# Nine output projections in three rounded passes, and fourteen middle taps added by DMA

## The chip, the cores and the metric

The kernel runs on one core of a Trainium2 chip. The metric is the device time of one execution in microseconds. Its engines are TensorE (PE; its weight loads are PEld), VectorE (DVE), ScalarE (ACT), GpSimd (POOL) and SyncE (SP), each with a queue of its own that it works through in order. They meet through semaphores.

## What is computed

A batch of 4 sequences of 1088 tokens goes through attention with a product of two sketches, then through a layer that mixes by a Fourier transform and has a small feed-forward part (layer 1), and then through layer 2, where the change is:

```python
h = np.maximum(x @ w_in, 0.0)                      # 128 -> 1024
hp = pad(h, 1, axis=1)
conv_out = sum(conv_w[k] * hp[:, k:k + S, :] for k in range(3))
gate = 1.0 / (1.0 + np.exp(-conv_out))
return h * gate @ w_out                            # 1024 -> 128
```

## The kernel before

Everything is fp32. Layer 2 keeps tokens in the free dimension: a chunk is one batch (of 4) and 128 of the 1024 hidden channels (of 8), so there are NI = 32 chunks, numbered i = 0 to 31 here, each 128 partitions by 1088 tokens. PSUM holds a chunk in three tiles of 364 columns.

A chunk goes through these steps, each on the engine that is named:

- `hidden(i)`, PE, L521 to L523: for each of three tiles, x times w_in in three passes. An fp32 value is split into a rounded high half (type fp32r) and the rest, the low half, and low x high, high x low and high x high are summed. The halves of x come from layer 1 (`x2hi`, `x2lo`).
- `relu(i)`, ACT, L792: three copies with relu from PSUM to `h2`, a ring of HIDDENS = 5 buffers. It waits for the product of chunk i - 5.
- `left_tap(i)` (L1056) and `right_tap(i)` (L1061), DVE: gate = ratio0 * left + middle, then gate = ratio1 * right + gate. The taps are scaled so that the middle one is 1; the sigmoid puts the scale back.
- `sigmoid(i)`, ACT, L798, in place in `gate`.
- `product(i)`, DVE, L1068: gate = h2 * gate.
- `project(i)`, PE, L600: three matmuls in fp32 with w_out (`wout`), which add up the eight chunks of a batch in three PSUM banks. `output(b)` (ACT, L807) copies them out after the eighth.

The order on each queue is written out. PE does hidden(i), then slots of layer 1, then the projections up to i + 1 - lag(i); `LAGS` sets how many chunks projection stays behind, 6 to 8. DVE does in its turn i left tap i, product i - 2 and right tap i. ACT does in its turn i relu i + 1, output if one is due, and sigmoid i - 1. Into all three a `slot(n)` of layer 1 is put where `PACES` says: up and down matmuls (L561 and others) on PE, `hidden_high` (L736) and `mixed_high` (L741) on ACT, low halves on DVE. The slots end at chunk 22. GpSimd works out the ten reciprocal deviations of layer 1 and has nothing to do later.

```python
LAGS = ((-1, 6), (15, 7), (19, 8), (24, 7), (26, 6), (28, 5), (30, 4))
def projected(i):
    return max(0, i + 1 - lag(i))
```

## Time and profile before

| | us |
|---|---|
| median of 3 runs | 256.98 (256.5 to 289.55) |
| the profiled execution | 256.51 |
| its span, first to last instruction | 254.7 |
| PE busy in it | 247.2 |
| DVE busy in it | 220.2 |
| ACT busy in it | 157.0 |

The span leaves out 1.8 us of the profiled execution's time that lie before the first and behind the last instruction. Busy time is the union of an engine's instructions; overlapping instructions of one engine count once.

### The profile page before, as it was taken

Reading aid. Unit: us, or ns where it says so; the run is one execution under the profiler, and the core shown is the slowest. Engines: PE = TensorE matmul, PEld = TensorE weight load, DVE = VectorE, ACT = ScalarE, POOL = GpSimd, SP = SyncE. Lnnn points to the kernel's source line nnn. Section 1 sums busy time; section 2 is a strip of 40 time slices with the busy share of each in tenths; the row PEclk is TensorE's granted clock in tenths of the full one; section 3 lists DMA queues with packets and bytes.
Section 4 is the critical chain, followed back from the end, with each engine's and each line's share of the span. In section 5 each row is a group of like instructions: output and inputs, shape, how many; then the busy total and the mean of one; then the engine's idle time right before and its main releaser. Section 6 shows DMA issues by size and latency. Waiting matters only on the chain.

```text
span 254.7 us, 4283 instructions
## 1 busy us (share of the span) xinstructions
PE 247.2 (97%) x1522; PEld 210.7 (83%) x1522; DVE 220.2 (86%) x404; ACT 157.0 (62%) x325; POOL 28.4 (11%) x90
## 2 busy tenths in 40 slices
PE   8999999999999999989999999999999999999995
PEld 7999999998989999978887777778778777777752
DVE  0847888899998688897799999999979999997992
ACT  2351733333586547688997766769769576667552
POOL 0000000001603343575200000000000000000000
PEclk9999999999999999999999999999999999999999
DMA  7959730300000000000000000002000002002002
GB/s 249 349 217 348 307 98 0 97 4 0 3 0 1 3 1 0 3 3 3 0 0 3 0 0 0 3 0 89 0 0 3 1 0 87 3 0 87 0 0 88
DMA packets 4340, 13.04 MB, mean 51 GB/s; under 512 B 736, under 2 KB 1504, under 8 KB 4320
## 3 DMA queue, kind: packets, MB, share of 16 engines
q1 hardware_dynamic: 4176, 12.74, 13.7%
q8 instruction: 12, 0.20, 0.3%
q14 instruction: 8, 0.07, 0.1%
q10 hardware_dynamic: 144, 0.03, 0.1%
HBM read 10.54 MB, written 2.23 MB: 50 GB/s over the span
## 4 chain that ended last, share of the span: by engine, by line
PE 46%; DVE 5%; ACT 3%; issue 2%; ACTq 0%
PE ps L600 20%; PE ps L521 7%; PE ps L523 7%; PE ps L522 7%; PE ps L561 5%; DVE arena L1061 2%; DVE arena L1056 1%; ACT arena L722 1%; ACT arena L798 1%; PE ps L552 1%; DVE arena L1068 1%; PE ps L531 0%; DVE x_nat L970 0%; DVE arena L977 0%; DVE x2lo L1004 0%
## 5 line engine op out<-in xcount | busy, mean ns | idle before, releaser
L600 PE MATMUL ps<-arena,wout 128*128 128x364 f32 (+1 forms) x192 | 62.8, 467 | 0.5 <-DVE arena L1068 0.5
L792 ACT ACTIVATE arena<-ps 128x364 f32<-128x364 f32 x96 | 42.6, 482 | 19.0 <-PE ps L523 16.8
L600 PEld LDWEIGHTS ps<-arena,wout 128*128 128x128 f32 x192 | 35.9, 189 | 20.6 <-issue 2.8
L1056 DVE SCALAR_TENSOR_TENSOR arena<-arena,ratio 128x1088 f32<-128x1088 f32 x32 | 43.1, 1346 | 1.9 <-ACT arena L792 1.9
L798 ACT ACTIVATE arena<-arena,base 128x1088 f32<-128x1088 f32 x32 | 38.8, 1211 | 7.3 <-DVE arena L1061 7.1
L1061 DVE SCALAR_TENSOR_TENSOR arena<-arena,ratio 128x1088 f32<-128x1088 f32 x32 | 43.1, 1346 | 0.1
L1068 DVE TENSOR_TENSOR arena<-arena 128x1088 f32<-128x1088 f32 (+2 forms) x36 | 41.3, 1159 | 1.5 <-ACT arena L798 1.3
L521 PE MATMUL ps<-x2hi,wlo 128*128 128x364 f32 x96 | 40.2, 419 | 0.7 <-ACT arena L736 0.4
L523 PE MATMUL ps<-x2hi,whi 128*128 128x364 f32 x96 | 31.5, 328 | 0.0
L522 PE MATMUL ps<-x2lo,whi 128*128 128x364 f32 x96 | 31.5, 328 | 0.0
L843 DVE TENSOR_TENSOR arena<-arena 109x1280 f32<-109x1280 f32 (+1 forms) x12 | 21.9, 1842 | 6.5 <-ACT arena L673 6.4
L521 PEld LDWEIGHTS ps<-x2hi,wlo 128*128 128x128 f32 x96 | 18.0, 188 | 5.8 <-ACT arena L792 1.8
L522 PEld LDWEIGHTS ps<-x2lo,whi 128*128 128x128 f32 x96 | 18.0, 188 | 3.8 <-issue 1.6
L448 PE MATMUL ps<-arena 121*128 121x66 f32 x144 | 18.6, 270 | 0.0
L722 ACT ACTIVATE arena<-x_nat,arena 109x128 f32<-109x128 f32 x40 | 16.4, 483 | 2.9 <-POOL arena L404 2.9
L523 PEld LDWEIGHTS ps<-x2hi,whi 128*128 128x128 f32 x96 | 18.0, 188 | 0.0
L673 ACT ACTIVATE arena<-ps 109x320 f32<-109x320 f32 (+2 forms) x16 | 6.7, 424 | 18.4 <-PE ps L436 16.0
L998 DVE SCALAR_TENSOR_TENSOR h1lo<-ps,h1hi 128x436 fp32r<-128x436 f32 x22 | 13.2, 604 | 5.5 <-ACT h1hi L736 5.5
L448 PEld LDWEIGHTS ps<-arena 121*128 121x128 f32 x144 | 17.7, 192 | 0.0
L479 PE MATMUL ps<-arena 128*109 128x66 f32 x160 | 17.1, 260 | 0.0
L436 PE MATMUL ps<-sketch,arena 128*109 128x64 f32 (+1 forms) x152 | 17.1, 266 | 0.0
L436 PEld LDWEIGHTS ps<-sketch,arena 128*109 128x109 f32 (+1 forms) x152 | 16.6, 184 | 0.2
(100 smaller groups left out, 404.2 us busy)
## 6 DMA issues: line engine op xcount, KB each, us to landing
arena<-v_d SPq DMA_DIRECT2D x4, 594.0 KB, 3.9
arena<-qT_d SPq DMA_DIRECT2D x3, 545.0 KB, 5.9
arena<-kT_d SPq DMA_DIRECT2D x3, 544.5 KB, 5.0
out_d<-arena SPq DMA_DIRECT2D x3, 544.0 KB, 2.7
cos_t<-cos_d SPq DMA_DIRECT2D x1, 926.5 KB, 5.9
sin_t<-sin_d SPq DMA_DIRECT2D x1, 926.5 KB, 7.7
arena<-qT_d SPq DMA_DIRECT2D x2, 272.5 KB, 3.8
wraw<-w_d SPq DMA_DIRECT2D x2, 256.0 KB, 5.1
```

What stands on the lines that cost most here:

```text
L436: mm = pe.matmul(ps[0:rows, bank_kq(n), c:c + H * AB], src[:, b % 2, t * rows:(t + 1) * rows], sketch[:], start=True, stop=True)
L448: mm = pe.matmul(ps[:, KV_BANK, pair * 2 * V1:(pair + 1) * 2 * V1], kphi[:, b % 2, t, 2 * pair:2 * pair + 2, :].rearrange("p h f -> p (h f)"),
L521: pe.matmul(out, lo, rhi, start=first, stop=False)
L522: pe.matmul(out, hi, rlo, start=False, stop=False)
L523: return pe.matmul(out, hi, rhi, start=False, stop=last)
L600: pe.matmul(ps[:, OUT_BANK + t, 0:z - a], wout[:, c, :], gate[:, i % GATES, a:z], start=(c == 0), stop=(c == C2 - 1)).then_inc(wout_done, 1)
L792: act.activation(h2[:, i % HIDDENS, t * TT:(t + 1) * TT], ps[:, bank_p(n), 0:TT], ACT.Relu).then_inc(h2_ready, 1)
L798: act.activation(gate[:, i % GATES, :], gate[:, i % GATES, :], ACT.Sigmoid, scale=base[:, i % C2:i % C2 + 1]).then_inc(gate_ready, 1)
L843: dve.tensor_tensor(phi.rearrange("p t h (i j) -> p (t h) i j", j=R), a, c, ALU.mult).then_inc(ready, 1)
L1056: dve.scalar_tensor_tensor(out=gate[:, i % GATES, :], in0=h2[:, i % HIDDENS, 0:S], scalar=ratio[:, 0, i % C2:i % C2 + 1], in1=h2[:, i % HI ...
L1061: dve.scalar_tensor_tensor(out=gate[:, i % GATES, :], in0=h2[:, i % HIDDENS, 2:S + 2], scalar=ratio[:, 1, i % C2:i % C2 + 1], in1=gate[:, ...
L1068: dve.tensor_tensor(gate[:, i % GATES, a:z], h2[:, i % HIDDENS, 1 + a:1 + z], gate[:, i % GATES, a:z], ALU.mult).then_inc(prod_ready, 1)
```

## The change

Of layer 2's 32 chunks, nine (`CAST` = 1, 4, 7, ... 25) get their projection in three rounded passes in place of fp32. For these, after the product, ACT copies the gate to fp32r (`product_high`, in its turn i + 2) and DVE subtracts that from the gate (`product_low`, in its turn i + LOW_LAG = i + 4). The halves have rings of three buffers. w_out is split once: a DMA from GpSimd's queue casts the high half, DVE subtracts the low one in its turn 3.

For fourteen chunks (`ADDED` = 2, 4, ... 28) DVE does no left tap. ACT copies ratio0 * left to the gate (`left_copy`, in its turn i - 1, behind relu i), a DMA from GpSimd's queue adds the middle tap to it in SBUF, and DVE's right tap i waits for that DMA and moves to the beginning of its turn i + 1.

GATES goes from 9 to 7 buffers, placed by `gate_places`; `LAGS` becomes 6 up to chunk 27, then 5 and 4. To make room, several buffers share memory that earlier stages have left (two of `h2` in `x_room`, two of the gate in `folded_room`), so names in the rows differ.

```diff
-GATES = 9
+ADDED = tuple(range(2, NI - 3, 2))
+CAST = tuple(range(1, NI - 4, 3))
+CASTS, LOW_LAG = 3, 4
+GATES = 7
 SPLIT_FROM = NI - 2
-LAGS = ((-1, 6), (15, 7), (19, 8), (24, 7), (26, 6), (28, 5), (30, 4))
+LAGS = ((-1, 6), (28, 5), (30, 4))
...
+        def gate_free(i):
+            last = max((n for n in range(i) if GATE_OF[n] == GATE_OF[i]), default=None)
+            if last is None:
+                return ()
+            return ((low_ready, CAST.index(last) + 1),) if last in CAST else ((wout_done, NT * (last + 1)),)
...
+            def cast_wout():
+                pool.wait_ge(ld_wout, 32)
+                pool.wait_ge(whi_ready, 3)
+                pool.wait_ge(wlo_ready, 3)
+                pool.dma_start(wout_hi[:], wout.rearrange("p c d -> p (c d)")).then_inc(wout_hi_ready, 16)
+
             for r in range(NR):
+                if r == 4:
+                    cast_wout()
...
+            def add_middle(n, i):
+                pool.wait_ge(copied, n + 1)
+                if n >= 2:
+                    pool.wait_ge(middle_added[n % 2], 16 * (n // 2))
+                pool.dma_start(gate(i), h2(i)[:, 1:S + 1], accum_op=ALU.add).then_inc(middle_added[n % 2], 16)
+
+            for i in ADDED:
+                add_middle(ADDED.index(i), i)
...
+                n = CAST.index(i) if i in CAST else None
+                if n == 0:
+                    pe.wait_ge(wout_lo_ready, 1)
+                if i in CAST:
+                    pe.wait_ge(high_ready, n + 1)
+                    pe.wait_ge(low_ready, n + 1)
                 for t in range(NT):
-                    pe.wait_ge(prod_ready, products(i, t))
+                    if i not in CAST:
+                        pe.wait_ge(prod_ready, products(i, t))
...
-                    pe.matmul(ps[:, OUT_BANK + t, 0:z - a], wout[:, c, :], gate[:, i % GATES, a:z],
+                    if i in CAST:
+                        w = slice(c * DM, (c + 1) * DM)
+                        three_pass(ps[:, OUT_BANK + t, 0:z - a], wout_hi[:, w], wout_lo[:, w], gate_hi[:, n % CASTS, a:z],
+                                   gate_lo[:, n % CASTS, a:z], c == 0, c == C2 - 1).then_inc(wout_done, 1)
+                        continue
+                    pe.matmul(ps[:, OUT_BANK + t, 0:z - a], wout[:, c, :], gate(i)[:, a:z],
...
+            def left_copy(i):
+                if i == ADDED[0]:
+                    act.wait_ge(ratios_ready, 2)
+                act.wait_ge(h2_ready, NT * (i + 1))
+                for free, count in gate_free(i):
+                    act.wait_ge(free, count)
+                act.activation(gate(i), h2(i)[:, 0:S], ACT.Copy,
+                               scale=ratio[:, 0, i % C2:i % C2 + 1]).then_inc(copied, 1)
...
+            def product_high(n, i):
+                act.wait_ge(prod_ready, i + 1)
+                for free, count in halves_free(n):
+                    act.wait_ge(free, count)
+                act.activation(gate_hi[:, n % CASTS, :], gate(i), ACT.Copy).then_inc(high_ready, 1)
...
+                    if i + 1 in ADDED:
+                        left_copy(i + 1)
                     for n in slots_b(i + 1):
                         slot(n)
...
                 if i >= 1:
                     sigmoid(i - 1)
+                if i - 2 in CAST:
+                    product_high(CAST.index(i - 2), i - 2)
...
             def right_tap(i):
-                dve.wait_ge(left_ready, i + 1)
+                if i in ADDED:
+                    n = ADDED.index(i)
+                    dve.wait_ge(middle_added[n % 2], 16 * (n // 2 + 1))
+                else:
+                    dve.wait_ge(left_ready, summed(i) + 1)
...
+            def product_low(n, i):
+                dve.wait_ge(high_ready, n + 1)
+                for free, count in halves_free(n):
+                    dve.wait_ge(free, count)
+                dve.tensor_tensor(gate_lo[:, n % CASTS, :], gate(i), gate_hi[:, n % CASTS, :].bitcast(F32),
+                                  ALU.subtract).then_inc(low_ready, 1)
...
             for i in range(NI + 2):
-                if i < NI:
+                if i - 1 in ADDED:
+                    right_tap(i - 1)
+                if i < NI and i not in ADDED:
                     left_tap(i)
...
                 if i >= 2:
                     product(i - 2)
-                if i < NI:
+                if i < NI and i not in ADDED:
                     right_tap(i)
+                if i == 3:
+                    wout_low()
+                if i - LOW_LAG in CAST:
+                    product_low(CAST.index(i - LOW_LAG), i - LOW_LAG)
```

The order of instructions at the places that the prediction speaks of follows. The first is VectorE from product 0 on. Before, product 0 (L1068), right tap 2, left tap 3, product 1, right tap 3:

```order
L1068 TENSOR_TENSOR arena<-arena 128x1088
L1061 SCALAR_TENSOR_TENSOR arena<-arena,ratio 128x1088
L1056 SCALAR_TENSOR_TENSOR arena<-arena,ratio 128x1088
L1068 TENSOR_TENSOR arena<-arena 128x1088
L1061 SCALAR_TENSOR_TENSOR arena<-arena,ratio 128x1088
```

Changed, from product 0 (L1167) to low half 1 (L1174); L1160 is the right tap, L1151 the left tap, L1179 the low half of w_out:

```order
L1167 TENSOR_TENSOR folded_room<-x_room,folded_room 128x1088
L1160 SCALAR_TENSOR_TENSOR arena<-arena,ratio 128x1088
L1151 SCALAR_TENSOR_TENSOR arena<-arena,ratio 128x1088
L1167 TENSOR_TENSOR folded_room<-x_room,folded_room 128x1088
L1160 SCALAR_TENSOR_TENSOR arena<-arena,ratio 128x1088
L1179 TENSOR_TENSOR wout_lo<-wout,wout_hi 128x1024
L1167 TENSOR_TENSOR arena<-arena 128x1088
L1160 SCALAR_TENSOR_TENSOR arena<-arena,ratio 128x1088
L1151 SCALAR_TENSOR_TENSOR arena<-x_room,ratio 128x1088
L1167 TENSOR_TENSOR arena<-arena 128x1088
L1160 SCALAR_TENSOR_TENSOR arena<-x_room,ratio,arena 128x1088
L1174 TENSOR_TENSOR gate_lo<-folded_room,gate_hi 128x1088
```

Left taps 2 and 4 are gone, right taps 2 and 4 stand where they stood or a place earlier, and the low half of w_out and low half 1 have come in.

The second is TensorE at projection 1, behind the last pass of hidden 7. Before, L600 is projection 1 and L521 begins hidden 8:

```order
L523 MATMUL ps<-x2hi,whi 128x364
L600 MATMUL ps<-arena,wout 128x364 x2
L600 MATMUL ps<-arena,wout 128x360
L521 MATMUL ps<-x2hi,wlo 128x364
L522 MATMUL ps<-x2lo,whi 128x364
```

Changed, L584 to L586 are the three passes, here of projection 1's first two tiles (the third has the same three with 360 columns, and then hidden 8 begins):

```order
L586 MATMUL ps<-x2hi,whi 128x364
L584 MATMUL ps<-gate_hi,wout_lo 128x364
L585 MATMUL ps<-gate_lo,wout_hi 128x364
L586 MATMUL ps<-gate_hi,wout_hi 128x364
L584 MATMUL ps<-gate_hi,wout_lo 128x364
L585 MATMUL ps<-gate_lo,wout_hi 128x364
L586 MATMUL ps<-gate_hi,wout_hi 128x364
```

The three fp32 matmuls have become nine passes in the same place, and the first waits for both halves of the gate.

The third is VectorE from product 26 on. Before, product 26 (L1068), right tap 28, left tap 29, product 27, right tap 29:

```order
L1068 TENSOR_TENSOR arena<-arena 128x1088
L1061 SCALAR_TENSOR_TENSOR arena<-arena,ratio 128x1088
L1056 SCALAR_TENSOR_TENSOR arena<-arena,ratio 128x1088
L1068 TENSOR_TENSOR arena<-arena 128x1088
L1061 SCALAR_TENSOR_TENSOR arena<-arena,ratio 128x1088
```

Changed, from product 26 (L1167) to left tap 30:

```order
L1167 TENSOR_TENSOR arena<-x_room,arena 128x1088
L1160 SCALAR_TENSOR_TENSOR arena<-arena,ratio 128x1088
L1151 SCALAR_TENSOR_TENSOR arena<-arena,ratio 128x1088
L1167 TENSOR_TENSOR folded_room<-arena,folded_room 128x1088
L1160 SCALAR_TENSOR_TENSOR arena<-arena,ratio 128x1088
L1174 TENSOR_TENSOR gate_lo<-arena,gate_hi 128x1088
L1151 SCALAR_TENSOR_TENSOR folded_room<-x_room,ratio 128x1088
```

Right tap 28 comes from turn 28 to the beginning of turn 29 with no other order of these instructions, since left tap 28 is gone; low half 25 (L1174) stands between right tap 29 and left tap 30. On TensorE, projection 25 follows hidden 30 in both, with projection 26 and hidden 31 behind it.

## Rows read from the trace of the kernel before

**Rows 1.** The page, busy time of each engine in the span.

```profile
PE 247.2 (97%) x1522; PEld 210.7 (83%) x1522; DVE 220.2 (86%) x404; ACT 157.0 (62%) x325; POOL 28.4 (11%) x90
```

**Rows 2.** Busy us by stretch: PE, PEld, DVE, ACT, POOL, clock, DMA share, GB/s.

```profile
141.00:204.00 63.00, 63.00 (x284) 48.96 (x283) 61.13 (x57) 46.01 (x85) 0.00 (x0) 1.00 0.03 10
204.00:246.00 42.00, 41.64 (x173) 30.46 (x172) 40.32 (x35) 28.27 (x48) 0.00 (x0) 1.00 0.07 27
```

**Rows 3.** The page's groups of instructions: busy, mean ns, idle before them.

```profile
L600 PE MATMUL ps<-arena,wout 128*128 128x364 f32 (+1 forms) x192 | 62.8, 467 | 0.5 <-DVE arena L1068 0.5
...
L792 ACT ACTIVATE arena<-ps 128x364 f32<-128x364 f32 x96 | 42.6, 482 | 19.0 <-PE ps L523 16.8
...
L798 ACT ACTIVATE arena<-arena,base 128x1088 f32<-128x1088 f32 x32 | 38.8, 1211 | 7.3 <-DVE arena L1061 7.1
```

**Rows 4.** Timeline of PE: start, us, line; projection 1, and the end of hidden 22.

```profile
140.94 2.00 PE L600 MATMUL ps<-arena,wout 128*128 128x364 f32 x6
...
142.94 0.33 PE L522 MATMUL ps<-x2lo,whi 128*128 128x364 f32 x1
...
203.82 0.89 PE L561 MATMUL ps<-arena,wraw 128*128 128x436 f32 x2
...
204.55 2.00 PE L600 MATMUL ps<-arena,wout 128*128 128x364 f32 x6
```

**Rows 5.** Timeline of DVE from product 0.

```profile
130.26 1.28 DVE L1068 TENSOR_TENSOR arena<-arena 128x1088 f32<-128x1088 f32 x1
131.46 1.35 DVE L1061 SCALAR_TENSOR_TENSOR arena<-arena,ratio 128x1088 f32<-128x1088 f32 x1
132.72 1.35 DVE L1056 SCALAR_TENSOR_TENSOR arena<-arena,ratio 128x1088 f32<-128x1088 f32 x1
133.99 1.28 DVE L1068 TENSOR_TENSOR arena<-arena 128x1088 f32<-128x1088 f32 x1
```

**Rows 6.** Timeline of ACT from relu 2 to relu 3.

```profile
124.61 1.19 ACT L792 ACTIVATE arena<-ps 128x364 f32<-128x364 f32 x3
125.71 0.54 ACT L736 ACTIVATE arena<-ps 128x436 f32<-128x436 f32 x1
126.44 0.67 ACT L741 ACTIVATE x2hi<-ps 128x218 fp32r<-128x218 f32 x3 [0.20 <-PE ps L561]
126.97 1.22 ACT L798 ACTIVATE arena<-arena,base 128x1088 f32<-128x1088 f32 x1
128.07 1.21 ACT L792 ACTIVATE arena<-ps 128x364 f32<-128x364 f32 x3
```

**Rows 7.** Timeline of PE from projection 22 to the end.

```profile
228.17 3.83 PE L600 MATMUL ps<-arena,wout 128*128 128x364 f32 x12
...
235.33 0.33 PE L522 MATMUL ps<-x2lo,whi 128*128 128x364 f32 x1
...
236.66 3.83 PE L600 MATMUL ps<-arena,wout 128*128 128x364 f32 x12
...
246.16 5.77 PE L600 MATMUL ps<-arena,wout 128*128 128x364 f32 x18 [0.52 <-DVE arena L1068]
```

**Rows 8.** Timeline of DVE: product 26, right tap 29, left tap 30.

```profile
233.63 1.29 DVE L1068 TENSOR_TENSOR arena<-arena 128x1088 f32<-128x1088 f32 x1 [1.35 <-ACT arena L798]
...
238.57 1.35 DVE L1061 SCALAR_TENSOR_TENSOR arena<-arena,ratio 128x1088 f32<-128x1088 f32 x1
...
239.83 1.35 DVE L1056 SCALAR_TENSOR_TENSOR arena<-arena,ratio 128x1088 f32<-128x1088 f32 x1
```

**Rows 9.** Timeline of ACT: output copies of batch 2, sigmoid 26.

```profile
230.87 1.63 ACT L807 ACTIVATE arena<-ps 128x364 f32<-128x364 f32 x3 [2.03 <-PE ps L600]
232.40 1.20 ACT L798 ACTIVATE arena<-arena,base 128x1088 f32<-128x1088 f32 x1
```

**Rows 10.** DMA issues: count, KB each, median us from issue to landing.

```profile
arena<-qT_d SPq DMA_DIRECT2D x3, 545.0 KB, 5.9
...
out_d<-arena SPq DMA_DIRECT2D x3, 544.0 KB, 2.7
```

94 lines of the change are left out of this document (65 added, 29 removed).

## The prediction

> **What bounds the kernel now.** I read the busy shares first, then the busy time by stretch, then the timeline of each engine at the two places where the change puts a new dependence. PE is busy 247.2 us of the 254.7 us span [rows 1]. By stretch it is busy for all 63 us from 141 to 204 and for 41.6 of the next 42 [rows 2]. The page's groups say the same from the other side: its projections, L600, waited 0.5 us in all [rows 3]. So TensorE sets the time. VectorE is almost a second bound: 61.1 of 63 us and 40.3 of 42 [rows 2]. ScalarE has room (46.0 of 63, 28.3 of 42), and it waits mostly for the others. A microsecond of TensorE work is worth a microsecond only if VectorE is in time with what TensorE asks for next. I number the 32 chunks of layer 2 from 0 and write projection 1, low half 1 and so on.
>
> **Durations.** From one start to the next, a tap costs VectorE 1.26 us and a product 1.20 [rows 5]. A ScalarE pass over 1088 columns costs 1.10 from start to start [rows 6] and ends 1.21 after its start [rows 3]. A low half is a two-operand pass like the product, so 1.20; the low half of wout has 1024 columns, 1.20 x 1024/1088 = 1.13.
>
> **Part 1, the rounded projections: -3.0 us.** Projection 1 starts at 140.94 and the second pass after it at 142.94; one pass of the next chunk lies between them [rows 4]. Eight three-pass matmuls run from 235.33 to 236.66, 0.167 us each [rows 7]. So a projection costs 2.00 - 0.17 = 1.83 us now and 9 x 0.167 = 1.50 in three passes. Nine of them save 9 x 0.33 = 3.0 us on the engine that bounds. Nothing else lies in this term, since the shapes are those of the hidden matmuls.
>
> **Part 2, VectorE and ScalarE in sum.** VectorE loses 14 left taps (17.6 us) and gains nine low halves (10.8) and one of wout (1.1): 5.7 us less. ScalarE gains 14 copies and nine high halves, 23 x 1.10 = 25.3 us. In the two stretches it had 17.0 + 13.7 = 30.7 us free [rows 2]. It stays under its limit, but gets late more often. By sums alone the change would gain 3.0 us. What decides is when each low half is ready, because TensorE takes its instructions in order: a projection that waits also holds the hidden matmuls behind it.
>
> **Part 3, projection 1: +4.8 us.** Projection 1 stands behind hidden 7 and starts at 140.94 [rows 4]. Now it needs low half 1, which VectorE does in its turn 5, behind right tap 5. From product 0 on VectorE had no gap here: 130.26, 131.46, 132.72 and 133.99 follow at once [rows 5]. From product 0 to the end of low half 1 there are now twelve instructions: products 0 to 3, right taps 2 to 5, left taps 3 and 5, the low half of wout and low half 1. That is 5 x 1.20 + 6 x 1.26 + 1.13 = 14.7 us. Beginning at 130.26 it ends at 144.95, 4.0 us after TensorE wants it. Product 0 comes later too. ScalarE has copy 2 between relu 2, which ends at 125.8, and the hidden copy that started at 125.71 [rows 6]. That pushes the hidden copy by 1.1 us, and the copies of x2 (126.44, which began after 0.20 us idle), sigmoid 0 (126.97) and relu 3 (128.07) stand behind it. By the starts that is 0.75 us for sigmoid 0 and all after it, since x2 could start at 127.2 and not at 126.4. Product 0 waits for the copy behind relu 3, so it moves by 0.75 as well. The wait is 4.8; its ends are 4.0 (copy 2 hidden) and 5.1 (all 1.1 passed on). The left taps 2 and 4 that VectorE loses can't help: product 0 was held by ScalarE, and the taps' room is counted above. After 141 TensorE has no idle time that could swallow this [rows 2].
>
> **Part 4, projection 19: +1.4 us.** In the last third there are no slots of layer 1 left, and chunks come fast. I count from the end of hidden 22. Relu 22 ends 0.5 us later (mean 482 ns [rows 3]), copy 22 at 1.6, sigmoid 20 at 2.8, product 20 at 4.0. The DMA that adds the middle tap lands at 1.6 + D. Right tap 22 starts at the later of 4.0 and 1.6 + D. Then come right tap 22, left tap 23, product 21, right tap 23 and low half 19: 3 x 1.26 + 2 x 1.20 = 6.2. TensorE meanwhile does projection 16 (1.5), the last slot (0.73, from 203.82 to 204.55 [rows 4]), hidden 23, 24 and 25 (4.5) and projections 17 and 18 (3.7), 10.4 in all. No row shows an adding DMA. The nearest two of its size land 2.7 us (a store out of SBUF) and 5.9 us (a load beside others) after issue [rows 10]. I take D = 4.0: nearer the store, which like it reads SBUF late in the program, with room for the second read that an addition needs. Right tap 22 then starts at 5.6 and low half 19 ends at 11.8: 1.4 us late. D = 2.7 gives 0.1, D = 5.9 gives 3.3. The Trainium skill, page "DMA: Bandwidth & Descriptors", section "Anatomy of one DMA", fits a DMA issued from GpSimd by 2.0 us plus bytes over 436 GB/s, so 3.3 us here without a price for the addition. By that estimate this wait would be 0.7 and the whole sum 6.4; the trace has no DMA from GpSimd to hold against it.
> Before this stage slots of layer 1 stretch the chunks: from 140.94 to 203.82 [rows 4] hidden 8 to 22 took 62.9 us, 4.2 each. Three chunks are 12.6 us against the 11.8 of the same chain, so projections 7 and 13 have 0.8 us to spare. Even low halves stand behind one product only and are early.
>
> **Part 5, projection 25 and the end: +3.9 us.** TensorE does projection 25 after hidden 30, at 236.66 [rows 7]. Low half 25 stands behind right tap 29, which in the trace of before only starts at 238.57 [rows 8]: the lag shrinks to 4 there, and the low half comes at 4 too. Product 26 starts at 233.63, after 1.35 us idle, because sigmoid 26 (232.40) stands behind the output copies of batch 2 (230.87), and these wait for projection 23 [rows 8, 9]. That stays, moved only by the 0.33 us that projection 22, ahead of it, saves. From product 26 come right tap 28, left tap 29, product 27, right tap 29 and now low half 25: the trace gives 239.83 - 233.63 = 6.2 for the five of before, which were the same, plus 1.2. Low half 25 ends at 233.63 - 0.33 + 7.4 = 240.7 on before's clock, and TensorE is there at 236.66 - 0.33 = 236.33. It waits 4.4 us. Hidden 31 stands behind it, and behind that the projections to the end, 11 us of TensorE work that VectorE now feeds in time; the 0.52 us that TensorE waited at 246.16 goes [rows 7]. Net +3.9. The least it can be is 5.4 us of latency from hidden 29 to low half 25 less the 3.3 of projection 24 and hidden 30, so 2.1 - 0.5 = 1.6.
>
> **Sum.** -3.0 + 4.8 + 1.4 + 3.9 = +7.1 us. On the profiled execution (256.5 us, 1.8 outside the span) that is 263.6, against a median of 256.98: 2.6% slower. I forecast 263.5. The terms' ends give 256.5 - 3.0 + 4.0 + 0 + 1.6 = 259.1 and 256.5 - 3.0 + 5.1 + 3.3 + 3.9 = 265.8.
> The GpSimd queue gets the cast of wout and 14 adds, the cast behind the statistics of unit 3 and the adds behind all ten; its own work stands idle between units, so I cost the issue at nothing. A copy that waits for its gate buffer (seven in place of nine) meets a used one only at copy 12, which waits for low half 7; VectorE has slack there.
>
> **The rivals.** (a) The first wait is there and the late ones shrink to their least, since TensorE, set back 4.8 us, gives VectorE time to run ahead: 256.5 - 3.0 + 4.8 + 1.6 = 259.9, and 261.3 with the 1.4 of projection 19. For it: VectorE has 5.7 us less to do. Against: the chains of parts 4 and 5 count from TensorE's own hidden matmuls and move with them. (b) The low halves come in time, because an engine's order is looser than I read it: then TensorE's saving stands, 256.5 - 3.0 = 253.5, at best 252. This is the other side. Its mechanism is VectorE's relief of 5.7 us, and it decides if low half 1 is done by 141, which needs VectorE 4 us ahead of where the trace has it. (c) The adding DMA is slow. At D = 6 the chain of part 4 is 13.8 us long: projection 19 waits 2.0 us more than in my sum, and projections 7 and 13 wait 1.2 each, 268 us. At D = 8 it is 4.0 more and 3.2 each, 274.
>
> **Chances.** The forecast (262 to 266) 0.5; (a) 0.26; (b) 0.10; (c) 0.14. The range leaves out (b) and the top of (c): 257.5 to 269. A measurement here can tell 2% from no change, so the bounds are 251.8 and 262.1. Faster: 0.03, the best of (b). Same: (a), the rest of (b) and a tail of the forecast, 0.37. Slower 0.60.
>
> **What would show it.** In the profile after: PE idle of 4 to 5 us before the first three-pass projection (or spread over the hidden matmuls just ahead), released by VectorE's low half; a smaller one at projection 19; one of 4 us at projection 25; PE busy about 3 us less; the last VectorE idle at the output copies still there. If PE shows no gap at projection 1, part 3 is wrong and (b) is near. If the adding DMAs land beyond 5 us, (c).

## The result: 7.2% slower, and the profile after

The changed kernel takes 275.1 us (mean of 273.9, 275.6 and 275.8), against 256.6 for the kernel before in runs taken beside it: the ratio is 1.072, interval 1.0668 to 1.0772. Some executions are longer by some 32 us (307 us for this kernel, 289 for the one before) and are left out of every comparison of times; the profiles of `only_rounds`, `low_turn_earlier`, `other_gate` and `lags_back` are of such executions, but the extra time lies ahead of layer 2, and from the first hidden matmul to the end `other_gate` takes 155.8 us there and the changed kernel 156.7, so their waits in layer 2 are read. The forecast was 263.5, range 257.5 to 269. The sign was right; the loss is 18.5 us (19.3 between the two profiled executions) where 7 were forecast.

The profiled execution took 275.77 us, its span is 274.0. The page of the changed kernel, busy time and clock by slices, against [rows 1]:

```profile
PE 252.5 (92%) x1549; PEld 219.6 (80%) x1549; DVE 215.9 (79%) x400; ACT 179.2 (65%) x348; POOL 41.5 (15%) x105
...
PEclk9999999999999999999979999999999996899599
```

PE should be busy about 3 us less, and it is busy 5.3 us more. Yet the rounded projections do save what they should (below). The clock line is the hint: in three places the granted clock is under full speed, which the page of before had nowhere. By stretch (columns as in [rows 2]: PE, PEld, DVE, ACT, POOL, clock, DMA share, GB/s):

```profile
126.00:140.00 14.00, 10.79 (x58) 9.03 (x57) 9.74 (x12) 13.09 (x25) 1.82 (x2) 0.99 0.41 80
140.00:150.00 10.00, 9.71 (x41) 7.65 (x40) 9.90 (x9) 8.56 (x14) 0.87 (x1) 0.84 0.30 57
...
220.00:230.00 10.00, 6.11 (x29) 4.97 (x28) 8.36 (x7) 7.75 (x13) 0.87 (x1) 0.92 0.52 100
230.00:240.00 10.00, 10.00 (x39) 8.64 (x37) 7.38 (x7) 6.98 (x10) 0.87 (x1) 0.74 0.18 36
...
250.00:260.00 10.00, 4.95 (x14) 4.16 (x15) 8.63 (x7) 2.13 (x4) 0.00 (x0) 0.66 0.00 0
```

Each stretch in which PE idles by several microseconds (126 to 140, 220 to 230, 250 to 255) is followed by one at a lower clock: 0.84, 0.74, 0.66 on average, a mixture of the levels 1.2 and 2.4 GHz.

Where PE waited, from the page's groups (L584 is the first pass of every three-pass product; the first row is the hidden matmuls, the second the rounded projections):

```profile
L584 PE MATMUL ps<-x2hi,wlo 128*128 128x364 f32 x96 | 38.8, 405 | 4.7 <-ACT arena L868 2.3
...
L584 PE MATMUL ps<-gate_hi,wout_lo 128*128 128x364 f32 (+1 forms) x27 | 11.1, 410 | 10.3 <-DVE gate_lo L1174 10.3
```

So the rounded projections waited 10.3 us for low halves, where the projections of before waited 0.5 [rows 3], and the hidden matmuls 4.7. The single waits, from the timeline of PE. First the beginning of layer 2 (hidden 4, hidden 6, projection 0 at L675, projection 1):

```profile
130.14 0.43 PE L584 MATMUL ps<-x2hi,wlo 128*128 128x364 f32 x1 [1.29 <-ACT arena L868]
...
138.37 0.43 PE L584 MATMUL ps<-x2hi,wlo 128*128 128x364 f32 x1 [1.92 <-ACT x_room L868]
...
140.20 3.44 PE L675 MATMUL ps<-folded_room,wout 128*128 128x364 f32 x6
...
146.75 0.41 PE L584 MATMUL ps<-gate_hi,wout_lo 128*128 128x364 f32 x1 [0.29 <-DVE gate_lo L1174]
...
148.32 0.33 PE L584 MATMUL ps<-x2hi,wlo 128*128 128x364 f32 x1
```

Projection 1 takes 148.32 - 146.75 = 1.57 us; projection 0, still fp32, takes 3.44 where six such records take 2.00 [rows 4]. Then projection 7 (172.83, 0.83 idle), projection 8 (177.58, 0.23, for the output copies), hidden 15 (180.66, 1.02), projection 13 (203.02, 0.24), and the two long waits, ahead of projections 19 and 25:

```profile
225.01 0.32 PE L586 MATMUL ps<-x2hi,whi 128*128 128x364 f32 x1
229.22 0.64 PE L584 MATMUL ps<-gate_hi,wout_lo 128*128 128x364 f32 x1 [3.89 <-DVE gate_lo L1174]
...
232.08 0.51 PE L584 MATMUL ps<-x2hi,wlo 128*128 128x364 f32 x1
...
234.81 1.61 PE L675 MATMUL ps<-folded_room,wout 128*128 128x364 f32 x4
...
255.05 0.64 PE L584 MATMUL ps<-gate_hi,wout_lo 128*128 128x364 f32 x1 [5.05 <-DVE gate_lo L1174]
...
257.90 2.62 PE L675 MATMUL ps<-arena,wout 128*128 128x364 f32 x6
```

Projection 19 runs from 229.22 to 232.08, 2.86 us where projection 1 took 1.57, and the nine passes of hidden 26 behind it take 2.73 where nine take 1.50 at full clock. Projection 20 takes 1.78 where projections at full clock take 1.56 from start to start. Projection 25 takes 2.85, and projection 26 2.19.

**The ledger**, span against span, 274.0 - 254.7 = 19.3 us. Idle time of PE ahead of these instructions is 13.9 us more than before (1.29, 1.92, 0.29, 0.83, 0.23, 1.02, 0.24, 3.89, 5.05, less the 0.33 and 0.52 of before). Matmuls at a lower clock cost 6.2: 1.4 at projection 0 and 0.2 in the passes just ahead of it, 2.7 at projection 19, hidden 26 and projection 20, 1.9 at projections 25 and 26. Each wait costs about 0.25 us beside its idle time (the first pass after 130.14 takes 0.27 in place of 0.167, and the last before a wait is followed to its end, 0.33 after its start, where the next one otherwise starts after 0.167); nine waits less the two of before make 1.8. The rounded passes save 3.0. Layer 1 ahead of all this ended 0.5 later in this execution (by as much as it differs from one execution to the next). That makes 13.9 + 6.2 + 1.8 - 3.0 + 0.5 = 19.4.

Now the chains behind the two long waits. DVE from product 20 on (L1167 product, L1160 right tap, L1151 left tap, L1174 low half 19):

```profile
219.87 1.29 DVE L1167 TENSOR_TENSOR folded_room<-x_room,folded_room 128x1088 f32<-128x1088 f32 x1
222.80 1.35 DVE L1160 SCALAR_TENSOR_TENSOR arena<-arena,ratio 128x1088 f32<-128x1088 f32 x1 [1.64 <-DMA arena<-arena]
...
227.79 1.28 DVE L1174 TENSOR_TENSOR gate_lo<-arena,gate_hi 128x1088 fp32r<-128x1088 f32 x1
```

and ACT from the output copies of batch 1 on (L898; then sigmoid, relu 22 at L868, x2, copy 22 at L876):

```profile
212.91 1.08 ACT L898 ACTIVATE arena<-ps 128x364 f32<-128x364 f32 x2
213.88 1.19 ACT L883 ACTIVATE arena<-arena,base 128x1088 f32<-128x1088 f32 x1
214.97 1.20 ACT L868 ACTIVATE arena<-ps 128x364 f32<-128x364 f32 x3
216.04 0.68 ACT L816 ACTIVATE x2hi<-ps 128x218 fp32r<-128x218 f32 x3
216.55 1.25 ACT L876 ACTIVATE arena<-arena,ratio 128x1088 f32<-128x1088 f32 x1
```

DVE from product 26 on, against [rows 8]:

```profile
246.81 1.29 DVE L1167 TENSOR_TENSOR arena<-x_room,arena 128x1088 f32<-128x1088 f32 x1
248.62 1.35 DVE L1160 SCALAR_TENSOR_TENSOR arena<-arena,ratio 128x1088 f32<-128x1088 f32 x1 [0.52 <-DMA arena<-arena]
...
253.62 1.28 DVE L1174 TENSOR_TENSOR gate_lo<-arena,gate_hi 128x1088 fp32r<-128x1088 f32 x1
```

The page's DMA issues (us from issue to landing), seven of the fourteen adds; the other groups of them read 4.7 too:

```profile
arena<-arena POOLq DMA_DIRECT2D x7, 544.0 KB, 4.7
```

### The profile page after: what moved, and what is told of

Same layout as the page of the kernel before. It is cut to its first block, busy times and chain, and to the rows that moved or that the text cites. A ratio compares the mean times of both kernels' runs of the same rounds, so it can differ in the third digit from the quotient of the medians.

```text
span 274.0 us, 4405 instructions
## 1 busy us (share of the span) xinstructions
PE 252.5 (92%) x1549; PEld 219.6 (80%) x1549; DVE 215.9 (79%) x400; ACT 179.2 (65%) x348; POOL 41.5 (15%) x105
## 4 chain that ended last, share of the span: by engine, by line
issue 40%; PE 8%; POOL 4%; ACT 3%; DVE 3%; DMA 2%; POOLq 0%; ACTq 0%; DVEq 0%
PE ps L675 4%; POOL arena L464 3%; DMA arena<-arena 2%; ACT arena L797 2%; PE ps L584 1%; POOL folded_room L464 1%; PE ps L586 1%; PE ps L585 1%; DVE arena L1160 1%; DVE arena L1151 0%; ACT arena L876 0%; DVE gate_lo L1174 0%; ACT arena L868 0%; PE ps L594 0%; ACT arena L811 0%
## 5 line engine op out<-in xcount | busy, mean ns | idle before, releaser
L584 PE MATMUL ps<-x2hi,wlo 128*128 128x364 f32 x96 | 38.8, 405 | 4.7 <-ACT arena L868 2.3
L586 PE MATMUL ps<-x2hi,whi 128*128 128x364 f32 x96 | 32.3, 336 | 0.0
L675 PE MATMUL ps<-arena,wout 128*128 128x364 f32 (+1 forms) x90 | 30.4, 475 | 0.0
L868 ACT ACTIVATE x_room<-ps 128x364 f32<-128x364 f32 x42 | 18.6, 476 | 13.6 <-PE ps L586 13.2
L584 PEld LDWEIGHTS ps<-x2hi,wlo 128*128 128x128 f32 x96 | 18.5, 192 | 9.6 <-ACT arena L868 3.8
L675 PEld LDWEIGHTS ps<-arena,wout 128*128 128x128 f32 x90 | 17.3, 194 | 9.8 <-issue 2.3
L868 ACT ACTIVATE arena<-ps 128x364 f32<-128x364 f32 x54 | 22.8, 493 | 1.2 <-PE ps L586 1.1
L585 PEld LDWEIGHTS ps<-x2lo,whi 128*128 128x128 f32 x96 | 18.5, 193 | 2.8 <-issue 1.1
L584 PE MATMUL ps<-gate_hi,wout_lo 128*128 128x364 f32 (+1 forms) x27 | 11.1, 410 | 10.3 <-DVE gate_lo L1174 10.3
L1160 DVE SCALAR_TENSOR_TENSOR arena<-arena,ratio 128x1088 f32<-128x1088 f32 x13 | 17.5, 1348 | 3.8 <-DMA arena<-arena 3.8
L1167 DVE TENSOR_TENSOR arena<-arena 128x1088 f32<-128x1088 f32 x13 | 16.7, 1286 | 2.6 <-ACT arena L883 2.6
L511 PE MATMUL ps<-attic,arena 121*128 121x66 f32 x144 | 18.6, 270 | 0.0
L586 PEld LDWEIGHTS ps<-x2hi,whi 128*128 128x128 f32 x96 | 18.5, 193 | 0.0
L675 PE MATMUL ps<-folded_room,wout 128*128 128x364 f32 (+1 forms) x48 | 17.7, 508 | 0.2 <-ACT arena L898 0.2
L511 PEld LDWEIGHTS ps<-attic,arena 121*128 121x128 f32 x144 | 17.7, 192 | 0.0
L499 PE MATMUL ps<-sketch,attic 128*109 128x64 f32 (+1 forms) x152 | 17.6, 272 | 0.0
L499 PEld LDWEIGHTS ps<-sketch,attic 128*109 128x109 f32 (+1 forms) x152 | 17.2, 189 | 0.2
```

Source lines behind the costliest of these rows:

```text
L499: mm = pe.matmul(ps[0:rows, bank_kq(n), c:c + H * AB], src[:, b % 2, t * rows:(t + 1) * rows], sketch[:], start=True, stop=True)
L511: mm = pe.matmul(ps[:, KV_BANK, pair * 2 * V1:(pair + 1) * 2 * V1], kphi[:, b % 2, t, 2 * pair:2 * pair + 2, :].rearrange("p h f -> p (h f)"),
L584: pe.matmul(out, lo, rhi, start=first, stop=False)
L585: pe.matmul(out, hi, rlo, start=False, stop=False)
L586: return pe.matmul(out, hi, rhi, start=False, stop=last)
L675: pe.matmul(ps[:, OUT_BANK + t, 0:z - a], wout[:, c, :], gate(i)[:, a:z], start=(c == 0), stop=(c == C2 - 1)).then_inc(wout_done, 1)
```

## The experiments

The theory after the result: (A) nearly all of the loss comes from low halves and high halves that stand in the order of DVE and ACT ahead of what TensorE needs, and from what TensorE's waits cost beyond their length. The rivals: (B) the adding DMAs and the right taps that wait for them; (C) ScalarE, which has 25 us more to do and paces the rest.

### The two halves of the change apart

Adds alone (`only_adds`; no rounded projection, no halves of w_out):

```diff
-CAST = tuple(range(1, NI - 4, 3))
+CAST = ()
...
-                if r == 4:
-                    cast_wout()
...
-                if i == 3:
-                    wout_low()
```

> The changed kernel with no rounded projections: no high and low halves, no split of w_out, all 32 projections in fp32; the 14 copies and adding DMAs, the 7 gate buffers and the lags stay. Theory A: nothing on TensorE waits for a low half, its work is that of the kernel before, 256 to 260 us. Theory B: all of the loss is still there, 270 us or more. Theory C: 14 of 23 added ScalarE passes stay, so most of the loss, 264 to 270 us.

Rounded projections alone (`only_rounds`):

```diff
-ADDED = tuple(range(2, NI - 3, 2))
+ADDED = ()
```

> The changed kernel with no adding DMAs: all left taps on VectorE as before, no ScalarE copies of them; the nine rounded projections stay. Theory A: each low half of an odd chunk stands behind still more VectorE work (14 left taps, 17.6 us in all), so TensorE waits more: 270 to 282 us. Theory B: the loss goes, 254 to 258 us. Theory C: only 9 of 23 added ScalarE passes stay, 256 to 262 us.

Adds alone: 1.0099 (1.0077 to 1.0121), 258.0 us in the profiled run. Rounds alone: 1.0807 (1.0777 to 1.0837), 276.3 us at best. Page of the adds alone:

```profile
PE 247.1 (96%) x1522; PEld 210.3 (82%) x1522; DVE 203.6 (79%) x390; ACT 170.8 (67%) x339; POOL 40.9 (16%) x104
```

Fourteen adding DMAs of 4.7 us each leave PE's busy time where it was and bring 1.3 us of wait at the start (hidden 4, behind copy 2; 0.33 before) and 0.6 more at the end. B falls, and so does C, which expected 264 us or more here and at most 262 for the rounds alone. The rounds alone keep the waits: 1.92 at hidden 6, 1.55 at projection 1, 0.95 at projection 4, 0.90 at hidden 15, 3.41 at projection 19, 4.44 at projection 25. The two last are 0.5 and 0.6 shorter than with the adds: that is what the adds, DMA and relieved left taps together, put on top of them. Yet the whole change is 2 us faster than the rounds alone. DVE is relieved (232.9 us busy against 215.9), but where the 2 us come from is not shown: the waits in the profile of the rounds alone add up to 1 us less than those of the changed kernel.

### What a wait of TensorE costs beyond its length

The ledger's clock term can be tested in the kernel before, which has neither halves nor adds. Projection 25 there is made to wait for a later product than its own, 28 (`before_wait`) or 27 (`before_wait_short`):

```diff
                 for t in range(NT):
+                    if i == 25:
+                        pe.wait_ge(prod_ready, products(28, 0))
```

> The kernel before with one wait added: projection 25 also waits for product 28, which ended at 242.4 in the trace while TensorE came to projection 25 at 236.7. One idle time of 5.7 us in TensorE and nothing else changed; hidden 31 stands behind it. If an idle microsecond costs a microsecond and no more: 256.5 + 5.7 - 0.5 (the wait at 246.2 that it swallows) = 261.7 us, or less if VectorE uses the time. If TensorE's granted clock falls after it as in the changed kernel (0.66 to 0.74 for some 5 us): 2 to 3 us more, 264 to 265 us.

> The kernel before with projection 25 also waiting for product 27, which ended at 238.7 with TensorE there at 236.7: one wait of about 2 us. If the clock falls after such a wait as it did after 5.6 us: 256.5 + 2.0 - 0.5 + 3 = 261 us. If a wait of 2 us costs only its length: 258 us. Projection 0 of the changed kernel, at half pace some 2 us after a wait of 1.9 us, speaks for part of the fall: 259 to 260 us.

With product 28 the ratio is 1.0322 (1.0281 to 1.0362), 8.3 us; with product 27 it is 1.0063 (1.0039 to 1.0087), 1.6 us. The profile of PE in the first, the wait and the twelve records behind it, and the stretches around it:

```profile
243.02 6.87 PE L602 MATMUL ps<-arena,wout 128*128 128x364 f32 x12 [5.62 <-DVE arena L1070]
```

```profile
237.00:242.00 5.00, 0.40 (x3) 0.10 (x1) 5.00 (x5) 1.98 (x3) 0.00 (x0) 1.00 0.00 0
242.00:247.00 5.00, 3.98 (x7) 2.36 (x8) 2.23 (x2) 0.00 (x0) 0.00 (x0) 0.52 0.00 0
247.00:252.00 5.00, 5.00 (x19) 3.55 (x18) 0.07 (x1) 1.53 (x4) 0.00 (x0) 0.80 0.00 0
```

and in the second:

```profile
238.18 3.93 PE L602 MATMUL ps<-arena,wout 128*128 128x364 f32 x12 [1.89 <-DVE arena L1070]
```

The same twelve records took 3.83 us before [rows 7]. After 5.6 us without work they take 6.87, at a granted clock of 0.52; after 1.9 us they take 3.93, and the clock reads 1.00 throughout. So in the profiled executions the long wait cost 3.0 us on top of its 5.6, and the short one 0.1. The short one isn't always so cheap: of its four executions three took 257.4 to 258.3 us at a mean clock of 1.00, and one took 259.05 at 0.992. Both ratios agree with that: either wait, a restart of 0.25, and the 0.52 that TensorE waits later in the kernel before [rows 7] and no longer does, 5.6 + 3.0 + 0.25 - 0.5 = 8.4 and 1.9 + 0.25 - 0.5 = 1.6.

The same question in the changed kernel (`warm_fill`): TensorE gets matmuls to do, whose results nobody reads, while it would wait at projections 19 and 25. They go into the bank of the next hidden tile, which is free.

```diff
+FILL = {19: (26, 20), 25: (31, 26)}
...
+                if i in FILL:
+                    spare_bank = bank_p(NT * FILL[i][0])
+                    ...
+                    for _ in range(FILL[i][1]):
+                        pe.matmul(ps[:, spare_bank, 0:TT], whi[:, 0:128], x2hi[:, 0, 0:TT], start=True, stop=True)
```

> The changed kernel with matmuls that compute nothing needed put into TensorE's two long waits: 20 passes of 364 columns (3.3 us) ahead of projection 19 and 26 (4.3 us) ahead of projection 25, into a PSUM bank that is free then. The waits for the low halves stay. If the slow clock behind the waits costs time of its own (it was granted at 0.74 in the 10 us behind the first, and projection 25 took 3.1 us in place of 1.5): 4 to 6 us less than the changed kernel's 275, so 269 to 271. If a wait costs only its own length: 275 us.

Measured 1.0548 (1.052 to 1.0576), 270.4 and 270.6 us: faster than the changed kernel by doing more work, 5.2 us between the profiled executions, 4.4 by the ratios. PE at projection 19 (L667 is the filling, 230.27 is hidden 26):

```profile
224.68 3.50 PE L667 MATMUL ps<-x2hi,whi 128*128 128x364 f32 x20
228.71 0.40 PE L585 MATMUL ps<-gate_hi,wout_lo 128*128 128x364 f32 x1 [0.54 <-DVE gate_lo L1181]
...
230.27 0.33 PE L585 MATMUL ps<-x2hi,wlo 128*128 128x364 f32 x1
...
231.77 1.99 PE L682 MATMUL ps<-folded_room,wout 128*128 128x364 f32 x6
```

Projection 19 begins 0.51 us before that of the changed kernel, which is the earlier start of layer 2 in this execution, so its low half came no sooner. It then takes 1.56 us in place of 2.86, and hidden 26 1.50 in place of 2.73. The clock reads 1.00 from 220 to the end. That shows the late part of the clock term: 2.5 us at projection 19, and from there to the end another 5.2 - 0.5 - 2.5 = 2.2, where the ledger has 0.2 at projection 20 and 1.9 at projections 25 and 26.

### Whose turn the low half has

A low half one turn earlier (`low_turn_earlier`):

```diff
-CASTS, LOW_LAG = 3, 4
+CASTS, LOW_LAG = 3, 3
```

> The changed kernel with each low half one VectorE turn earlier (turn i+3 in place of i+4). Theory A (TensorE stands in order behind low halves that come late, and its clock falls after each long wait): for odd chunks the low half then stands behind one product in place of two taps, a product and a tap, about 5 us earlier, so the waits at projections 7, 19 and 25 (0.8, 3.9 and 5.1 us) and the slow clock behind them go: 256 to 261 us. Theory B (the adding DMAs and the right taps that wait for them are the cause): they are untouched, 270 us or more. Theory C (ScalarE has 25 us more to do and paces the rest): untouched as well, 270 us or more.

Measured 1.034 (1.0315 to 1.0365), 264.8 and 265.2 us, 4 beyond the expectation's upper end, but 10 us less than the changed kernel, for each of nine DVE instructions one turn earlier. The waits for low halves fall from 10.3 us to 2.0 (0.60 and 1.42, at projections 22 and 25); left are those of the hidden matmuls (1.29 and 1.91 at the start, 0.90, 0.69) and 2.1 for products near the end. So the low half's place decides the two long waits, and the start is another matter. The edit also changes the order in which gate buffers are given out; `other_gate` (below) shows for another such order that it moves nothing.

### The start, the end, the gate buffers and the lag

`start_as_before` begins both edits at chunk 4, `no_last_cast` leaves chunk 25 in fp32, and `other_gate` lets no left copy wait for a low half by giving out the gate buffers otherwise:

```diff
-ADDED = tuple(range(2, NI - 3, 2))
-CAST = tuple(range(1, NI - 4, 3))
+ADDED = tuple(range(4, NI - 3, 2))
+CAST = tuple(range(4, NI - 4, 3))
```

> The changed kernel with projection 1 in fp32 and the left tap of chunk 2 on VectorE: no copy 2, no high half 1, no low half 1. The prediction's term for this place was 4.8 us; the trace shows waits of 1.3, 1.9 and 0.3 us there against 0.3 before, and projection 0 took 1.2 us longer at a low clock, with 0.33 us given back. If the place costs what it shows, and the later waits keep their size: 4 to 5 us less than the changed kernel, 270 to 271 us. If the later waits grow by what is gained here, since VectorE then has less time: 273 to 275 us.

```diff
-CAST = tuple(range(1, NI - 4, 3))
+CAST = tuple(range(1, NI - 7, 3))
```

> The changed kernel with eight rounded projections, 25 back in fp32. Its wait of 5.1 us and the slow clock behind it go (some 3 us), and 0.33 us of TensorE work and the 0.5 us wait at the end come back: 266 to 268 us. If the low half were not the cause, and TensorE would wait there for the output copies or for ScalarE: 272 us or more.

```diff
-until[place] = i + LOW_LAG if i in CAST else next(...)
+until[place] = i + LOW_LAG + 1 if i in CAST else next(...)
```

> The changed kernel with only the placement of the gate buffers changed: a buffer whose last user is a rounded chunk counts as free one turn later, so that copy 12 takes the buffer of chunk 5 and not that of chunk 7. If ScalarE's wait of 4.25 us at copy 12 for low half 7 hurts: TensorE's 1.0 us wait before hidden 14 and part of the later ones go, 271 to 273 us. If there is slack, as the prediction said: 275 us.

- `start_as_before`: 1.0518 (1.0497 to 1.0539), 269.1 to 269.9. Only 0.33 is waited at the start, as before; the later waits keep their sizes (0.92, 3.90, 5.09). It is faster than the changed kernel by 5.2 us by the ratios, 5.5 by the means and 6.7 between the two profiled executions. The place of projection 1 gives 5.3 for the start itself: it begins 5.8 later than before [rows 4], 0.5 of it from layer 1. In the profiled execution another 1.7 comes from the clock behind the late waits: after 3.90 us it fell only two passes into projection 19 and was back within hidden 26, 1.5 us lost in place of 2.7, and after 5.09 us 1.4 in place of 1.9. So waits of one length don't always cost the same. Without roundings, leaving out the add of chunk 2 is worth 1.9 us (1.0099 against 1.0024 for `adds_from_4`, below).
- `no_last_cast`: 1.0525 (1.0498 to 1.0552), 269.5 to 270.3. The wait of 5.05 and its slow clock go, and a wait of 1.13 us for a product comes instead close to the end, which the expectation (266 to 268) had not: the net is 5.0 by the ratios.
- `other_gate`: 1.0726 (1.0689 to 1.0764), as the changed kernel. ScalarE waits 4.25 us at copy 12 for low half 7 in the changed kernel (below) and not at all here, and TensorE's waits stay (0.85, 0.90, 3.88, 5.04).

```profile
172.78 1.21 ACT L876 ACTIVATE folded_room<-arena,ratio 128x1088 f32<-128x1088 f32 x1 [4.25 <-DVE gate_lo L1174]
```

The change also took two gate buffers and the longer lag of projection. `lags_back` gives both back, with halves in rings of two, and `lags_low3` has besides the low half a turn earlier:

```diff
-CASTS, LOW_LAG = 3, 4
-GATES = 7
-LAGS = ((-1, 6), (28, 5), (30, 4))
+CASTS, LOW_LAG = 2, 4        # lags_low3: 2, 3
+GATES = 9                    # two of them in a tensor of their own
+LAGS = ((-1, 6), (15, 7), (19, 8), (24, 7), (26, 6), (28, 5), (30, 4))
```

> The changed kernel with the lags of before (up to 8 chunks in the middle) and nine gate buffers again, for which the rings of halves have two buffers in place of three. Projection 19 then stands two chunks later, some 6.6 us against its low half's 3.7 us of lateness. If the shorter lag is what makes that wait: the 3.9 us wait and the slow clock behind it (2.6 us) go, projections 1 and 25, with lags as before, keep theirs: 267 to 269 us. If not: 275 us.

> The same, and each low half one turn earlier (turn i+3). Both ways of giving the low halves time together; the version of the low halves alone took 264.8 us. Its remaining waits at projections 22 and 25 (0.6 and 1.4 us) should shrink, those at the start stay (ScalarE's copy 2 ahead of relu 3, and the high half 1 ahead of relu 5, which waits for product 1): 261 to 264 us.

`lags_back` 1.0476 (1.0449 to 1.0503), 268.0 to 269.9; `lags_low3` 1.0227 (1.0211 to 1.0243), 262.0 to 262.7. With the lags of before, projection 19 follows hidden 26 and doesn't wait, where it waited 3.89, while projection 25, which follows hidden 30 in both, still waits 4.45. With both, no wait for a low half over 0.25 us is left.

The start of `lags_back` settles a question of the ledger. It has the same two waits as the changed kernel, 1.29 us at hidden 4 and 1.92 at hidden 6, but the clock stayed at 1.00. Hidden 6, projection 0 and projection 1:

```profile
170.47 0.44 PE L585 MATMUL ps<-x2hi,wlo 128*128 128x364 f32 x1 [1.92 <-ACT x_room L869]
...
172.08 1.99 PE L676 MATMUL ps<-folded_room,wout 128*128 128x364 f32 x6
...
178.85 0.40 PE L585 MATMUL ps<-gate_hi,wout_lo 128*128 128x364 f32 x1 [1.96 <-DVE gate_lo L1175]
```

Projection 0 takes 1.99 us here and 3.44 in the changed kernel, but projection 1 then waits 1.96 for low half 1 where it waited 0.29. From the start of hidden 4 to that of projection 1 both take 16.61 us. So the low clock at the start cost nothing: it ran in time that TensorE would have waited.

### Which chunks: is there a version that gains?

`even_casts` rounds chunks 4, 10, 16 and 22 with the rest of the change as it is; `adds_from_4` has the adds alone from chunk 4 on; three more stand on `lags_low3`:

```diff
 # even_casts
+CAST = tuple(range(4, NI - 8, 6))
 # adds_from_4 (on only_adds)
+ADDED = tuple(range(4, NI - 3, 2))
 # mid_lags (on lags_low3)
+ADDED = tuple(range(6, 24, 2))
+CAST = (7, 10, 13, 16, 19)
 # few_late_adds (on lags_low3)
+ADDED = (22, 24, 26, 28)
+CAST = (10, 13, 16, 19)
 # more_late_adds (on lags_low3)
+ADDED = (18, 20, 22, 24, 26, 28)
+CAST = (10, 13, 16, 19, 21, 23)
```

> The changed kernel with only four rounded projections, those of chunks 4, 10, 16 and 22, whose low halves stand behind one product and not behind two taps, a product and a tap. Theory A (waits for low halves): no wait but small ones, TensorE's work less by 4 x 0.33 = 1.3 us against the kernel with the adds alone (258.0 to 258.8): 256.5 to 258.5 us. If four rounded projections cost in proportion to nine, whatever their place, 4/9 of the way from 258 to 275: 265 us.

> The version with the adds alone (258.0 to 258.8 us), without copy 2: middle taps by DMA for chunks 4, 6, ... 28. If copy 2 pushing sigmoid 0 and relu 3 makes TensorE's 1.3 us wait ahead of hidden 4 (0.3 before): about 1 us less than that version, 257 to 257.6. If the loss of that version lies elsewhere: no change, 258.5 us.

> Lags of before, nine gates, low halves in turn i+3, and only the middle of the program changed: rounded projections 7, 10, 13, 16 and 19, middle taps added by DMA for chunks 6, 8, ... 22. Start and end are those of before, where ScalarE and the low halves made TensorE wait. If all loss comes from these two places and TensorE is full in the middle: 5 x 0.33 = 1.65 us less than before, 255 us (ratio 0.994). If the extra ScalarE work or the adding DMAs cost something in the middle too: 257 us or more.

> Rounded projections 10, 13, 16 and 19 with low halves in turn i+3, lags of before, and middle taps by DMA only for chunks 22, 24, 26 and 28, behind the slots of layer 1. TensorE has 4 x 0.33 = 1.3 us less to do. If ScalarE's copies between the slots ate the gain of the middle version: ratio 0.995 to 0.997, about 255.3 us. If a wait of VectorE or ScalarE at the end paces the kernel anyway: 256.5 us.

> Six rounded projections (10, 13, 16, 19, 21, 23) and middle taps by DMA for 18, 20, ... 28: TensorE has 2.0 us less. If the gain grows with the number of rounded projections: ratio 0.992 to 0.995. If low halves 21 and 23, where no slot stretches the chunks, come late again: 257 us or more.

| | ratio, interval | waits of PE in layer 2 that before has not |
|---|---|---|
| even_casts | 1.0123 (1.0097 to 1.0148) | 1.0 at the start, 0.91, 1.71 at projection 22, 0.4 |
| adds_from_4 | 1.0024 (1.0014 to 1.0034) | 0.6 at the end |
| mid_lags | 1.0007 (0.9994 to 1.0019) | 0.91 |
| few_late_adds | 1.0059 (1.0042 to 1.0076) | 0.91, 0.33, 0.2 at the end |
| more_late_adds | 1.0055 (1.0033 to 1.0076) | 0.91, 0.66, 0.41, 1.1 at the end |

None beats the kernel before, and the last three were expected to (by 0.3 to 0.8%); `even_casts` was expected at 258.5 us at most and took 258.9 to 260.1. The best, `mid_lags`, has PE busy 245.7 us, 1.5 less than before as its five rounded projections should, and a span of 254.8 against 254.7. Its one wait of note is at hidden 15, for relu 14. ACT there, in this kernel:

```profile
170.56 1.21 ACT L899 ACTIVATE arena<-ps 128x364 f32<-128x364 f32 x3
171.62 1.23 ACT L884 ACTIVATE arena<-arena,base 128x1088 f32<-128x1088 f32 x1
172.72 1.14 ACT L891 ACTIVATE gate_hi<-folded_room 128x1088 fp32r<-128x1088 f32 x1
173.72 1.23 ACT L869 ACTIVATE arena<-ps 128x364 f32<-128x364 f32 x3
```

and in the kernel before:

```profile
170.40 1.21 ACT L807 ACTIVATE arena<-ps 128x364 f32<-128x364 f32 x3
171.45 1.23 ACT L798 ACTIVATE arena<-arena,base 128x1088 f32<-128x1088 f32 x1
172.55 1.23 ACT L792 ACTIVATE arena<-ps 128x364 f32<-128x364 f32 x3
```

Output copies of a batch, sigmoid, relu: the three are in a row behind a projection in both, and TensorE is waiting for the relu. The high half has been put between sigmoid and relu, so the relu begins 173.72 - 172.55 = 1.17 us later and TensorE stops for 0.91 us. The same wait of 0.90 to 1.02 is in every version that rounds chunk 10, and not in the two that round nothing. Against the kernel before it sets hidden 15 back by 0.9 us, half of the 1.65 that five rounded projections give. The order that would cure it (the high half behind relu 14) was not run. Another 0.55 us goes at hidden 8, whose relu 7 begins at 142.63 in place of 141.40. Left copy 6 isn't the cause: `few_late_adds` has no copy there, and its relu 7 begins at 142.76, behind a sigmoid that waits 2.02 us for a right tap. It is the low half of w_out in DVE's turn 3, which these versions keep (in `few_late_adds`):

```profile
136.67 1.22 DVE L1180 TENSOR_TENSOR wout_lo<-wout,wout_hi 128x1024 fp32r<-128x1024 f32 x1
```

`adds_from_4`, which has copies 4 and 6 but no halves of w_out, starts relu 7 at 140.89. No version with this low half at another place was run.

## Why the prediction was wrong

By its own terms, in microseconds of PE's time against the kernel before (the measured column takes the waits with 0.25 each for the restart; the loss between the two profiled executions is 19.3):

| | forecast | measured |
|---|---|---|
| part 1, rounded passes | -3.0 | -3.0 |
| part 3, to projection 1 | +4.8 | +5.3 |
| projections 7, 8 and 13, hidden 15 | 0 | +3.3 |
| part 4, projection 19 | +1.4 | +4.1, and 2.7 of clock |
| part 5, projection 25 and the end | +3.9 | +4.5, and 1.9 of clock |
| layer 1 | 0 | +0.5 |
| sum | +7.1 | +19.3 |

- **Two steps failed. They make 5.8 and 4.8 of the missing 12.2 us.** The first: an idle microsecond was counted as one microsecond. The second: the chain of part 4 was taken as too short (output copies and the copies of x2 on ScalarE left out, the adding DMA at 4.0 us), and the waits at projections 7 and 13, and at hidden 15 behind a high half, were put at nothing.
- **The first step.** Every term turned a length of wait straight into time. There was no term for the clock, since the profile of before has no wait long enough to show one [rows 2]. Matmuls behind the waits of 3.89 and 5.05 us lost 2.7 and 1.9 us to a lower clock. The runs that show it: in the kernel before, a wait of 5.6 us costs 8.6 and one of 1.9 hardly more than itself; with TensorE kept at work the changed kernel is 4.4 to 5.2 us faster. The clock makes 4.6 of the missing 12.2 us, and five restarts of 0.25 us that no term had make 1.2 more. The rest is longer waits: 2.5 at projection 19, 2.3 at projections 7, 8 and 13 and hidden 15, 0.6 at projection 25, 0.5 at the start, and 0.5 of layer 1, which is no part of the change.
- **The second step, part 4: 1.4 forecast, 3.9 idle.** TensorE's 10.4 us from the end of hidden 22 to projection 19 came out exact (215.0 to 225.3). The chain on the other side was 14.1 us, not 11.8. Two terms of it: copy 22 ended 2.8 after hidden 22 and not 1.6, because the output copies and a sigmoid stood ahead of relu 22 (214.97, in the rows above) and the copies of x2 (216.04) between it and copy 22, and D was 5.0 and not 4.0: from the copy's end at 217.8 to right tap 22 at 222.80, of which the issue takes 0.3 to begin and the DMA 4.7. The fit that I set beside it (the Trainium skill, "DMA: Bandwidth & Descriptors", "Anatomy of one DMA") gives an estimate of 3.3 us for it, without a price for the addition; the trace has 4.7. Rival (c), a slow DMA, so had part of this term right, but the adds alone cost 2.5 us in all: it isn't the cause of the loss. The shorter lag, which the change brought, is what leaves projection 19 no room: with the lags of before it doesn't wait.
- **The second step, projections 7 and 13: said to have 0.8 us to spare.** Projection 7 waited 0.83 and projection 13 0.24. The chain of part 4 was taken at 11.8 us against 12.6 of TensorE, a margin smaller than its error (it took 14.1 at chunk 19). What the prediction didn't look at there is the high half ahead of a relu: hidden 15 waited 1.02 for relu 14, which began at 180.07 behind the high half at 179.07. It costed ScalarE by sums (25 us into 30 free) and said that ScalarE "gets late more often", without following which relu.
- **Part 3: right in size, wrong in place.** Low half 1 was to end 14.7 us after product 0 begins. It ended 14.8 after (131.80 to 146.60), and projection 1 began 5.3 us late apart from layer 1's 0.5. But only 0.29 of this showed as a wait for the low half. TensorE had lost the rest before: 1.29 at hidden 4, whose relu 3 stands behind copy 2, and 1.92 at hidden 6, whose relu 5 (137.86) stands behind high half 1, and that waited for product 1 (0.82 idle on ACT). It then lost 1.6 at low clock, which cost nothing, as `lags_back` shows: at full clock TensorE waited so much longer for low half 1. The prediction allowed for waits "spread over the hidden matmuls just ahead", and its sum held, since DVE's chain sets the end of all of them.
- **Part 5: the mechanism as foretold.** Product 26 began late behind the output copies of batch 2 (sigmoid 26 at 245.58), TensorE came to projection 25 3.03 us after it (249.84; by the prediction's numbers 236.33 - 233.30 = 3.03), and low half 25 ended 8.1 us after product 26 began, not 7.4: the 0.52 us that right tap 28 waited for its DMA, and the low half's end 1.28 after its start where I had counted 1.20. The 0.52 us of TensorE near the end did go, and its restart with it.
- **Part 1** is right: 1.57 us with the restart for projection 1, 1.50 for nine passes. PE's busy time rose all the same, because busy time counts matmuls at half clock as long ones.
- **Copy 12** has the slack that was claimed: it waits 4.25 us, and taking the wait away changes nothing. Likewise the queue of GpSimd: it stood idle for 4.8 us or more ahead of each add.
- **The rivals.** (b), the other side, was not near: no version that was run is faster than the kernel before. (a) would have needed the late waits to shrink as TensorE is set back; they didn't, as the case against it said, because the chains count from TensorE's own hidden matmuls. `start_as_before` shows this from the other side: with the first wait gone the late ones are 3.90 and 5.09, as large as ever.

What stays open is when a wait costs clock, and how much. It did after each of the eleven waits of 3.4 us or more in these profiles, but by 1.4 to 3.0 us, and not in the order of their lengths (1.4 after 5.09, 2.7 after 3.89). After waits of 1.9 us it did or didn't. Eight kernels have such a wait at hidden 6. In seven of them the clock fell behind it, for 1.6 us or so, also in `only_rounds`, where the wait at hidden 4 is only 0.32 (projection 0 takes 3.46 us there). In the eighth, `lags_back`, it didn't, with the same 1.29 and 1.92 as in the changed kernel, nor did it in the profiled execution of `before_wait_short`. Executions of one kernel differ too: the three of the changed kernel took 275.8, 275.6 and 273.9 us at mean clocks of 0.969, 0.969 and 0.981. So the length of the last wait alone doesn't decide it, and the clock terms above are those of the profiled executions.

## What to carry to other kernels

When an edit puts a new step ahead of an in-order engine that is the bound, don't ask whether the helper engines have room in sum; write down the chain from the last thing the bound engine delivers to the first it will ask for, with every instruction that stands ahead in each queue, and compare it with what the bound engine has to do meanwhile, place by place. Here DVE was relieved of 4.3 us and TensorE of 3, and 19 were lost, ten of which came back by doing one kind of DVE instruction, the low half, a turn earlier. The TensorE waits of 3.4 us and more were dearer here than their length in the profile, and `warm_fill` made two of them cheaper by keeping TensorE at work; look for the same when a kernel has waits of that order.
